# The first chunk's order of work in a fused recurrence and two-layer kernel: gates, clears, spreads and fillers

## The reference

```
# gated recurrence, B=2, H=8 (16 heads), S=768, D=40, per step t
m_new = max(f[t] + m, i[t]);  fs = exp(f[t] + m - m_new);  is_ = exp(i[t] - m_new);  m = m_new
C = fs*C + is_ * v k^T ;  n = fs*n + is_ * k
y[t] = sigmoid(o[t]) * (C q) / max(|n . q|, 1)
# then, x = y as 1536 tokens x 320
x = (h - tanh(h)) @ w_out1,            h = x @ w_in1    # 320 -> 2048 -> 320
x = (h * tanh(softplus(h))) @ w_out2,  h = x @ w_in2    # 320 -> 2048 -> 320
```

## Time and profile before

| | |
|---|---|
| median of 3 runs | 439.61 us (438.23 to 439.62) |
| the profiled execution | 439.19 us |
| its span, first to last instruction | 437.4 us |
| first matmul of layer 1 | 19.38 us |
| PE busy | 428.3 us (98%) |
| ACT, DVE, POOL busy | 277.9, 267.5, 162.9 us |

### The profile page before, as it was taken

How to read it: one execution, slowest core, us unless ns; L and a number is a source line. 1 busy time by engine, 2 the same in 40 slices (tenths; PEclk the granted TensorE clock), 3 DMA queues, 4 the chain that set the end, 5 groups by cost and what they waited for, 6 DMA issues and landing times.

```text
span 437.4 us, 9502 instructions
## 1 busy us (share of the span) xinstructions
PE 428.3 (98%) x3501; PEld 416.8 (95%) x3501; DVE 267.5 (61%) x547; ACT 277.9 (64%) x480; POOL 162.9 (37%) x130
## 2 busy tenths in 40 slices
PE   8998989999999999999999999999999999999997
PEld 5898979999999999999999999999999999999996
DVE  6866894587559476735636665675755564565460
ACT  5977447326524642542347589898788779777991
POOL 3456804220422222142219325434541452254243
PEclk9999999999999999999999999999999999999999
DMA  6992500160024015500053030000000000000001
GB/s 211 294 304 79 176 25 1 52 201 1 21 84 144 0 49 177 165 2 1 0 146 121 0 121 1 1 11 23 0 31 0 0 30 0 0 30 2 1 0 61
DMA packets 14861, 28.10 MB, mean 64 GB/s; under 512 B 1584, under 2 KB 7472, under 8 KB 14832
## 3 DMA queue, kind: packets, MB, share of 16 engines
q1 hardware_dynamic: 14444, 26.72, 19.7%
q10 hardware_dynamic: 388, 0.99, 0.8%
HBM read 25.71 MB, written 2.00 MB: 63 GB/s over the span
## 4 chain that ended last, share of the span: by engine, by line
PE 81%; DVE 8%; ACT 6%; issue 3%; POOL 1%; POOLq 1%; DVEq 0%; ACTq 0%
PE bank L1107 37%; PE bank L1115 32%; PE bank L1075 4%; PE bank L1048 2%; DVE act_lo L222 2%; PE bank L1060 2%; PE bank L1091 1%; DVE act L838 1%; ACT act_hi L525 1%; PE bank L1085 1%; ACT act_hi L639 1%; PE bank L1240 1%; ACT soft L626 1%; PE bank L1157 1%; ACT soft L631 1%
## 5 line engine op out<-in xcount | busy, mean ns | idle before, releaser
L1107 PE MATMUL bank<-x_lo,wi_hi 128*128 128x256 f32 x528 | 141.8, 283 | 0.0
L1115 PE MATMUL bank<-wo_hi,act_hi 128*128 128x320 f32 x384 | 119.9, 312 | 1.0 <-DVE act_lo L222 0.7
L1115 PE MATMUL bank<-wo_hi,act_lo 128*128 128x320 f32 x384 | 118.6, 309 | 0.0
L1115 PE MATMUL bank<-wo_lo,act_hi 128*128 128x320 f32 x384 | 118.6, 309 | 0.0
L461 POOL TENSOR_TENSOR act_lo<-hid,act_hi 128x512 fp32r<-128x512 f32 x48 | 66.6, 1417 | 97.9 <-ACT act_hi L639 97.9
L1107 PE MATMUL bank<-x_hi,wi_hi 128*128 128x256 f32 x352 | 101.7, 289 | 0.6 <-DVE x_lo L832 0.6
L1107 PEld LDWEIGHTS bank<-x_lo,wi_hi 128*128 128x128 f32 x528 | 101.1, 192 | 0.0
L1107 PE MATMUL bank<-x_hi,wi_lo 128*128 128x256 f32 x352 | 99.6, 283 | 0.0
L222 POOL TENSOR_TENSOR act_lo<-act,act_hi 128x512 fp32r<-128x512 f32 x28 | 36.0, 1287 | 120.6 <-ACT act_hi L525 120.6
L1115 PEld LDWEIGHTS bank<-wo_hi,act_hi 128*128 128x128 f32 x384 | 72.3, 188 | 2.2 <-POOL act_lo L461 1.1
L1115 PEld LDWEIGHTS bank<-wo_lo,act_hi 128*128 128x128 f32 x384 | 72.3, 188 | 0.0
(11 more groups left out here) (126 smaller groups left out, 661.4 us busy)
## 6 DMA issues: line engine op xcount, KB each, us to landing
stage<-w_out SPq DMA_DIRECT2D x8, 640.0 KB, 6.5
decay<-neg_top_rows SPq DMA_DIRECT2D x8, 512.0 KB, 3.8
stage<-w_in SPq DMA_DIRECT2D x6, 512.0 KB, 7.4
ks<-k_t SPq DMA_DIRECT2D x12, 160.0 KB
kt<-k_tok SPq DMA_DIRECT2D x6, 320.0 KB, 5.4
out<-out_sb SPq DMA_DIRECT2D x12, 160.0 KB, 1.8
v<-v_tok SPq DMA_DIRECT2D x5, 328.0 KB, 4.8
qs<-q_t SPq DMA_DIRECT2D x10, 160.0 KB
```

The costliest lines, as they stand in the source:

```text
L1107: last = pe.matmul(dst, w, x, start=(n == 0), stop=(n == len(parts) - 1))
L1115: last = pe.matmul(dst[b][:, 0:DM], a[:, t], w[:, j, :], start=(first and n == 0), stop=(last_tile and n == 2))
```

## The change

It touches the prologue alone, and one place in the first `steps`.

- SP loads gf first, with a semaphore of its own; `scan_sums(0, 0)` waits for it alone, `scan_maxima(0)` for gi.
- The clear of qs is halved between POOL (heads' first half) and DVE (second half).
- POOL clears the state after the v load and the ones column, no longer at the end of the constants; DVE waits for that clear before `update_state`, not before its first copy.
- PE's fillers between the spreads and inside the sums go; the scores of heads 0 to 7 come before the spread of q = 3; the turn of chunk 1's first column goes behind the state sums; the spread of chunk 1's q = 1 goes behind the second turn of y, and that of q = 0 into the first layer-1 tile, beside q = 2 and 3.
- ACT computes chunk 1's gate exponentials before the sigmoid, no longer after `split_high` of unit 0.
- DVE does `split_top(1)` and the copy of chunk 1's first column between the two `x_low`, no longer before the first `mix`.

```diff
@@ -151,9 +151,9 @@
 
 
     c_pool, c_dve = s("constants_pool"), s("constants_dve")
-    filler_ready, qs_clear = s("filler_ready"), s("qs_clear")
-
-    gates0_in = s("gates0_in")
+    filler_ready, qs_clear, qs_clear_dve = s("filler_ready"), s("qs_clear"), s("qs_clear_dve")
+
+    gates0_in, forget0_in = s("gates0_in"), s("forget0_in")
     gates2_in = s("gates2_in")
     gates_in, qk_in, flat_in = s("gates_in"), s("qk_in"), s("flat_in")
     kt_in, v_in, og_in = s("kt_in"), s("v_in"), s("og_in")
@@ -340,8 +340,8 @@
                 sp.wait_ge(sums, 2 * c - 1 + half)
                 sp.dma_start(decay[:, n, :], flat[n, :].partition_broadcast(P)).then_inc(spread[half], 16)
 
-        for dst, src in ((gi, gate_i), (gf, gate_f)):
-            sp.dma_start(dst[:, 0:2, :], src[0:2].rearrange("a h t -> h a t")).then_inc(gates0_in, 16)
+        sp.dma_start(gf[:, 0:2, :], gate_f[0:2].rearrange("a h t -> h a t")).then_inc(forget0_in, 16)
+        sp.dma_start(gi[:, 0:2, :], gate_i[0:2].rearrange("a h t -> h a t")).then_inc(gates0_in, 16)
         for odd in range(2):
             sp.dma_start(ks[odd * ODD:odd * ODD + D, :, :],
                          k_t[bass.ds(0, 1), odd].rearrange("a d h t -> (a d) h t")).then_inc(qk_in, 16)
@@ -397,7 +397,7 @@
         pool.memset(causal[:, :], 0.0).then_inc(pool_link, 1)
         pool.memset(pick[:, :].bitcast(F32), 0.0).then_inc(pool_link, 1)
         pool.wait_ge(pool_link, 3)
-        pool.memset(qs[32:ODD, :, :], 0.0).then_inc(qs_clear, 1)
+        pool.memset(qs[32:ODD, 0:HP // 2, :], 0.0).then_inc(qs_clear, 1)
         pool.wait_ge(qs_clear, 1)
         pool.affine_select(out=ident[:, :], in_=ident[:, :], compare_op=ALU.not_equal, fill=1.0, base=0,
                            pattern=[[-1, P]], channel_multiplier=1).then_inc(c_pool, 1)
@@ -411,13 +411,15 @@
         pool.wait_ge(c_pool, 5)
         pool.tensor_copy(pick[32:32 + NH, :], ident[32:32 + NH, 32:32 + NH]).then_inc(c_pool, 1)
         pool.wait_ge(c_pool, 6)
-        pool.memset(state[:, :, :], 0.0).then_inc(c_pool, 1)
         pool.sem_inc(lows, RING)
 
         def weigh_keys(c, first):
             if first:
                 pool.wait_ge(v_in, 16)
                 pool.memset(v1[:, :, D:E], 1.0).then_inc(v_ones, 1)
+                pool.wait_ge(v_ones, 1)
+                pool.memset(state[:, :, :], 0.0).then_inc(c_pool, 1)
+                pool.wait_ge(c_pool, 7)
             else:
                 pool.wait_ge(v_in, 16 * (c + 1))
             pool.wait_ge(cols_ready, c + 1)
@@ -579,6 +581,7 @@
         act_.wait_ge(filler_ready, 1)
         act_.activation(spark[:, :], filler[:, 0:1], ACT.Exp).then_inc(act_link, 1)
         act_.wait_ge(qs_clear, 1)
+        act_.wait_ge(qs_clear_dve, 1)
         for odd in range(2):
             act_.dma_start(qs[odd * ODD:odd * ODD + D, :, :],
                            q_t[bass.ds(0, 1), odd].rearrange("a d h t -> (a d) h t")).then_inc(qk_in, 16)
@@ -590,9 +593,9 @@
         weights_of(0, 0)
         weights_from_rows(0, 2)
         weights_from_rows(0, 3)
+        gate_exponentials(1, 1)
         output_gate(0, NB)
         split_high(act_, 0)
-        gate_exponentials(1, 1)
         act_.wait_ge(c_dve, 1)
         for b in range(NB):
             x_high(y_turned, acc, b, b + 1, y_high)
@@ -699,7 +702,7 @@
         def scan_sums(c, slot, buf=0):
 
             if c in (0, 1) if isinstance(c, int) else False:
-                dve.wait_ge(gates0_in, 32)
+                dve.wait_ge(forget0_in, 16)
             elif slot == 0:
                 dve.wait_ge(gates2_in, 32)
                 dve.wait_ge(gate_rows, 1)
@@ -855,6 +858,7 @@
         dve.sem_inc(last_low, 1)
         dve.memset(m_new[:, :], NEG).then_inc(dve_link, 1)
         dve.memset(ones[:, :], 1.0).then_inc(dve_link, 1)
+        dve.memset(qs[32:ODD, HP // 2:HP, :], 0.0).then_inc(qs_clear_dve, 1)
         for n in range(2):
             dve.memset(rows[n][:, :], 0.0).then_inc(dve_link, 1)
         for n in range(2):
@@ -862,9 +866,10 @@
         dve.memset(low_half[0:REM, :], 0.0).then_inc(dve_link, 1)
         dve.memset(low_half[REM:P, :], 1.0).then_inc(c_dve, 1)
         links[0] = 7
-        scan_gates(0, 0)
+        scan_sums(0, 0)
+        dve.wait_ge(gates0_in, 16)
+        scan_maxima(0)
         split_top(0)
-        dve.wait_ge(c_pool, 7)
         dve.wait_ge(a_turned, 1)
         dve.tensor_copy(cols[:, 0:NH], inter[:, 0:NH]).then_inc(a_cols, 1)
         dve.wait_ge(a_cols, 1)
@@ -873,16 +878,17 @@
         scan_maxima(1, 1)
         weigh_scores(0, 0)
         weigh_scores(0, 1)
-        dve.wait_ge(a_turned, 2)
         gate_columns(0, True)
         weigh_scores(0, 2, acc)
         weigh_scores(0, 3, acc)
-        split_top(1)
-        dve.tensor_copy(cols[:, 0:NH], inter[:, 2 * P:2 * P + NH]).then_inc(a_cols, 1)
         for b in range(NB):
             mix(0, b, True)
-        for b in range(NB):
-            x_low(acc, b, y_high, b + 1, x_ready)
+        x_low(acc, 0, y_high, 1, x_ready)
+        split_top(1)
+        dve.wait_ge(a_turned, 2)
+        dve.tensor_copy(cols[:, 0:NH], inter[:, 2 * P:2 * P + NH]).then_inc(a_cols, 1)
+        x_low(acc, 1, y_high, 2, x_ready)
+        dve.wait_ge(c_pool, 7)
         for b in range(NB):
             update_state(0, b, True)
         gate_columns(1, False, 1)
@@ -1163,7 +1169,7 @@
 
             if first and (k, slot) == (0, 0):
                 pe.wait_ge(x_ready, 2)
-                for q in (2, 3):
+                for q in (0, 2, 3):
                     mask_rows(1, q)
                     spread_rows(1, q)
             if (k, slot) == (0, 3 if first else 1):
@@ -1249,41 +1255,38 @@
         pe.wait_ge(filler_ready, 1)
         keep_dense(6)
         pe.wait_ge(c_pool, 4)
-        for q in range(1, NQ):
-            mask_rows(0, q)
+        mask_rows(0, 1)
+        mask_rows(0, 2)
         turn_first_column(0, inter[:, 0:NH])
-        keep_dense(1)
         pe.wait_ge(top_split, 1)
         pe.wait_ge(c_pool, 6)
-        for q in ORDER:
-            spread_rows(0, q)
-            if q != 1:
-                keep_dense(1)
+        spread_rows(0, 1)
+        spread_rows(0, 0)
         pe.wait_ge(a_cols, 1)
         turn_gates(0, True)
+        spread_rows(0, 2)
         scores_of(0, 0, 0, True)
         scores_of(0, 0, 1, True)
-        turn_first_column(1, inter[:, 2 * P:2 * P + NH])
-        keep_dense(1)
+        mask_rows(0, 3)
+        spread_rows(0, 3)
         scores_of(0, 1, 0, True, acc)
         scores_of(0, 1, 1, True, acc)
+        keep_dense(1)
         for b in range(NB):
             for part in range(2):
-                keep_dense(1)
                 sum_chunk(0, b, part, True)
         keep_dense(1)
+        turn_y(0, 0, True)
         for b in range(NB):
             sum_state(0, b)
-        keep_dense(1)
-        turn_y(0, 0, True)
+        pe.wait_ge(cols_ready, 1)
+        turn_first_column(1, inter[:, 2 * P:2 * P + NH])
+        keep_dense(2)
+        turn_y(0, 1, True)
+        keep_dense(2)
+        mask_rows(1, 1)
         pe.wait_ge(top_split, 2)
-        mask_rows(1, 1)
         spread_rows(1, 1)
-        keep_dense(1)
-        turn_y(0, 1, True)
-        pe.wait_ge(sums_read, 2)
-        mask_rows(1, 0)
-        spread_rows(1, 0)
         turn_gates(1, True)
         steps(0, 1, 2, True)
         with pe.Fori(1, G - 2) as g:
```

## The result

The changed kernel took 448.25 us, the median of 4 runs (447.74 to 448.89), against 439.48 (438.23 to 439.62) for the kernel before beside it: ratio 1.0209, interval 1.0195 to 1.0224. That is 8.8 us slower, where 1.9 were forecast, and outside the range of 438.4 to 442.8. Repeated on another chip it took 448.29, ratio 1.0211 (1.0194 to 1.0228). One thing must be known to read the numbers: a share of the executions of most kernels here, 21 of 89 of the kernel before, take about 449 us (the one that was profiled, 449.88 us of `e10_full_q0_back`, runs its prologue at the 1.2 GHz pace throughout), and the comparisons leave these out, while the changed kernel took 447.4 to 448.9 in all eight executions.

What follows compares the result with a forecast made beforehand. PE was taken as the bound, busy 428.3 of 437.4 us. Layer 1 1.27 later plus 0.62 for the q = 0 spread made 1.9; 439.19 + 1.9 = 441.1 us, own range 440.2 to 442.2, stated range 438.4 to 442.8.

Steps and rivals of the forecast that it cites:

- up to the second y: Prologue from the start to the second y: earlier by 1.25 us, at 15.95 in place of 17.20.
- worth little: DVE is now the bound here: At the normalisation: two of 1.88 us in a row on DVE set the second y, so removing fillers gains little.
- the cold-clock rival: Prologue and first layer-1 tiles: clock falls to 1.2 GHz in PE's idle 17.3 to 19.8, 2 us more, 443; chance 0.11.
- the wait for the queries: Ahead of chunk 0's scores: possible at 6.8, queries land at 7.3; scores start there in place of 8.30, 1.0 gained.
- The sign given for a cold clock: At layer 1's start: matmuls with starts 0.24 us apart at first in place of 0.12.
- The port step: Second y to layer 1: both DVE split operations wait for POOL's subtractions; layer 1 at 20.65, 1.27 later than 19.38.
- The table reload: ACT before chunk 1's weights: 1.28 us moves behind x_hi, 16.65 to 17.95, hidden by a wait; weights start at 20.35.
- The early start: Start of the prologue: gf first and state cleared later make the split maxima ready at about 4.50 in place of 5.54.
- The spread of q = 0: First layer-1 tile: mask and spread, hidden before, add 0.62 us until tanh can start.
- Moves rigidly to the end: After the prologue: weight units 3 to 7 come off DMA in time; what comes later moves rigidly, PE 1.9 us late.

Runs made afterwards that it cites:

- e10_full_q0_back: Changed kernel with removed fillers restored, split operations ahead of the first normalisation, chunk 1's q = 0 mask and spread ahead of layer 1 again: 440.43 us, ratio 1.0027.
- e7_split_early_only: Changed kernel with both split operations of chunk 1 ahead of the first normalisation, no fillers restored: 447.16 us, ratio 1.0178.
- e12_spread_fillers: Changed kernel with early split operations and fillers around the spreads, four of them in the wait for the queries, none in the sums: 440.14 us, ratio 1.0041.
- e1_fillers: Changed kernel with all removed fillers restored where they stood: 443.40 us, ratio 1.0101.
- e2_sum_fillers: Changed kernel with fillers restored in the sums alone, not between the spreads: 449.28 us, ratio 1.023.
- e11_before_split_late: Kernel before with chunk 1's split operations and column copy between the two x_low, q = 1 spread behind y's second turn, three fillers ahead of it: 442.62 us, ratio 1.0084.
- e14_table_ahead: e12_spread_fillers with a one-column exponential on ACT behind the first high part, to move the table reload into idle time: 440.23 us, ratio 1.0027.
- e9_before_gates_clears: Kernel before with only forget gates first, the clear of qs halved between POOL and DVE, and the state cleared later: 439.37 us, ratio 1.0004.
- e15_table_ahead_q0_back: e14_table_ahead with chunk 1's q = 0 mask and spread ahead of layer 1 again: 440.21 us, ratio 1.0036.
- e4_full_split_early: Changed kernel with all fillers restored, three more in the wait for the queries, split operations ahead of the first normalisation: 440.6 us, ratio 1.0047.
- e3_before_no_fillers: Kernel before without its eight fillers behind the first turn, between the spreads and inside and between the sums: ratio 1.0007.
- e13_act_order_back: e12_spread_fillers with chunk 1's gate exponentials on ACT back behind the sigmoid, the log and the first high part: 440.19 us, ratio 1.0031.
- e17_table_ahead_wait_filled: e14_table_ahead with seven fillers ahead of PE's wait near 43 us: 442.65 us, ratio 1.0077.
- e16_query_wait_only: Changed kernel with early split operations and four fillers, all in the wait for the queries: executions of 439.63, 442.14, 449.0 and 448.9 us.

## Why the prediction was wrong

- **The failed step** is the sentence in "up to the second y" that the fillers are "worth little: DVE is now the bound here", and with it the price and place of the cold-clock rival: chance 0.11, 2 us, in PE's idle time from 17.3 to 19.8. In the changed kernel the fall came at 7.7 us, behind the wait for the queries. The forecast itself had worked this wait out (the scores could start at 6.8, the queries land at 7.3), without asking what it does to the clock once the fillers around it are gone. From there PE's small matmuls ran at half pace, PE became the bound (DVE waits 2.44 and 1.53 in the rows above), and the second y came at 21.78 in place of 15.95. Price: 7.0 us (`e7_split_early_only` to `e12_spread_fillers`; 6.0 by the ratios), or 4.8 with the slow split operations still there (the changed kernel to `e1_fillers`). That the missing fillers make the prologue cold is shown; that the wait is what sets it off is not, since `e7_split_early_only` was cold without one. The sign given for a cold clock, layer-1 matmuls 0.24 apart, did not show: the clock was back when layer 1 began.
- The rule of the Trainium skill that the prediction named beside that rival is in TensorE: Matmul & The Clock Gate, "HAM oscillation — how this bites in real kernels": idle gaps make the clock fall. Both profiles of the changed kernel agree in kind, with a wait of 0.82 and 0.96 us ahead of the fall; `e7_split_early_only` and `e2_sum_fillers`, cold without a wait, show that it is not the whole.
- **The port step was right in kind**: both split operations waited, the first for the end of POOL's first half and the second for that of the other. The sum took 3.8 for the pair, and 3.4 was found (1.57 and 1.79 us). `e11_before_split_late` prices it at 3.3 us at the end.
- **The table reload**, 0 in the sum as "covered by the wait for `top_split`", was a second failed step. The order shown ahead of the prediction has the load waiting for `a_cols`, which DVE's copy sets, behind the split operations. So it came at 25.87, and chunk 1's weights, which set the end, at 27.16 and not at 26.3, when PE's spread was there. Taken out of the way it gave 0.9 us at the weights and 1.2 at the end (`e12_spread_fillers` to `e14_table_ahead`, profiled executions).
- **The early start** gave 0.6 of the 1.04 us forecast at the split maxima (4.92, forecast 4.50, before 5.53): their operations take 0.21 and 0.28, but DVE's clears now end at 2.69, where the sum was to start at 2.4 to 2.5. In `e12_spread_fillers` the second y stands at 16.58, 0.6 earlier than before, not 1.25; in `e1_fillers` and `e9_before_gates_clears` it stands as before.
- **The spread of q = 0**, 0.62 in the sum: moving it back moves no median (`e10_full_q0_back` 440.43; `e15_table_ahead_q0_back` against `e14_table_ahead`). PE's start is not what sets the end.
- **"Moves rigidly to the end"** was right, but from chunk 1's weights on and not from layer 1's start: 8.5 us at the weights, 8.5 at the end of the wait for `decay`, 8.6 at 81 us. The stretch at 0.66 after 50 us adds about 0.1.

That the change is slower was forecast, and about 3 of the 8.8 us come from the step that was to make it so; the larger part has another cause.

The sum as found: 4.85 for the clock of the prologue (448.25 - 443.40), 3.11 for the split operations beside POOL (443.40 - 440.29, the mean of two executions), 0.81 for the rest (440.29 - 439.48), near the 0.9 of the table reload; together 8.77. What the third term consists of is read from profiles; no run brings the median of a kernel with the change down to the kernel before.

## What to carry to other kernels

Matmuls whose result nobody reads are part of the schedule: before they are removed or work is moved ahead of a load, list the waits and the long rows of small matmuls that PE will then have, and price a low clock over everything up to the next dense stretch, not over the gap alone. Profile more than one execution: the same list can lose its clock at two places or never have it. An early start that ends in a wait for a transfer is worth nothing unless the transfer moves too. Put short DVE operations with operands in SBUF ahead of the event that releases POOL's long ones; here each one that came behind waited for the end of a POOL instruction, whatever its own size. Look for the row that the end follows, here ACT's first weights of the next chunk, before pricing the start of the engine that is busiest.

## What the runs showed of the hardware

- In the two profiles of the changed kernel the granted clock fell to 1.2 GHz at 7.7 and 8.9 us, 0.2 and 1.1 us behind a wait of 0.82 and 0.96, and stayed there for 17 and 14 us although the rows show PE busy nearly throughout: busy with scores and sums.
- The same list up to the sums can also start cold and stay so: in `e7_split_early_only` and `e2_sum_fillers` PE kept the 1.2 GHz pace (8 spreads in 1.97 us) to 22.8 and 26.5 us, without a wait ahead of the scores.
- Single fillers among small matmuls did not lift a low clock (`e2_sum_fillers`, and `e10_full_q0_back` at 449.88 us with all of them); behind four in a row it was high (`e4_full_split_early`, scores in 1.16 us behind spreads in 1.98).
- Behind 32 sums without a filler the clock fell for 3.4 us in four profiles (`e3_before_no_fillers`, `e13_act_order_back`, `e15_table_ahead_q0_back`, `e17_table_ahead_wait_filled`) and held in three others (`e12_spread_fillers`, `e14_table_ahead`, `e16_query_wait_only`).
- A DVE operation of 16 x 128 elements in SBUF took 1.57 and 1.79 us beside POOL's pair of 3.57, and 0.21 and 0.28 elsewhere. The two engines alternated instruction by instruction: neither got two in a row in the changed kernel, in `e1_fillers` or in `e11_before_split_late`.
- A fall of the clock for 3.4 to 6.8 us behind the wait near 44 us (52 in the changed kernel) cost 0.0 to 0.14 us; one at 58.4 us, in the kernel with that wait filled, cost 0.8.
